# Second MoE of an attention and MoE chain: units of two tiles with 256-column first-layer products and two sets of split second weights

## The reference

```python
logits = x @ w_gate                       # 3072 x 8
expert_idx = np.argmax(logits, axis=1)
probs = softmax(logits)
gate_w = probs[np.arange(N), expert_idx]
for e in range(E):                        # E = 8
    mask = expert_idx == e
    xe = x[mask]
    h = np.maximum(xe @ w1[e], 0.0)       # 512 -> 1024
    ye = h @ w2[e]                        # 1024 -> 512
    out[mask] = gate_w[mask, None] * ye
```

## Time and profile before

| | us |
|---|---|
| median of 3 runs (lowest, highest) | 483.22 (481.46, 484.78) |
| the profiled execution, device time | 484.04 |
| its span, first to last instruction | 482.3 |
| PE busy | 454.6 (94%) |
| DVE busy | 235.2 (49%) |
| ACT busy | 226.3 (47%) |
| POOL busy | 203.1 (42%) |

### The profile page before, as it was taken

One profiled execution on the slowest core, in us unless ns is written; L12 is line 12 of the kernel. 1 busy time (PEld: TensorE's weight loads), 2 busy tenths in 40 slices (PEclk: granted clock), 3 DMA queues, 4 the chain that ended last, 5 costly groups with the idle time before them and its releaser, 6 DMA issues. The chain is left out here.

```text
span 482.3 us, 9916 instructions
## 1 busy us (share of the span) xinstructions
PE 454.6 (94%) x3215; PEld 380.6 (79%) x3216; DVE 235.2 (49%) x760; ACT 226.3 (47%) x455; POOL 203.1 (42%) x179
## 2 busy tenths in 40 slices
PE   8899999999999979989999997999999999999972
PEld 7689999999999976734445864788888888888852
DVE  6567777777777743453210685423333332333352
ACT  2588778878788625321100007333344343334441
POOL 3998888888888100101000000043333333333322
PEclk9999999999999989997998979899999999999977
DMA  8699898976772139479991094511111111111111
GB/s 247 262 419 365 316 378 319 362 246 221 260 256 82 47 98 410 196 269 389 399 408 63 6 379 151 180 54 54 38 49 54 49 54 54 54 40 47 51 29 28
DMA packets 27156, 89.06 MB, mean 185 GB/s; under 512 B 3248, under 2 KB 3248, under 8 KB 27120
## 3 DMA queue, kind: packets, MB, share of 16 engines
q1 hardware_dynamic: 23664, 78.47, 43.9%
q0 software_dynamic: 3296, 9.70, 6.0%
q10 hardware_dynamic: 160, 0.42, 0.4%
HBM read 80.72 MB, written 8.13 MB: 184 GB/s over the span
## 5 line engine op out<-in xcount | busy, mean ns | idle before, releaser
L438 ACT ACTIVATE Pb<-Pb,nm 128x256 f32<-128x256 f32 (+1 forms) x192 | 83.9, 486 | 32.8 <-DVE nm L541 32.8
L381 PE MATMUL O<-V,PTs 128*128 128x65 f32 x704 | 90.1, 269 | 1.0 <-ACT PTs L464 1.0
L1357 PE MATMUL Gp<-w2h,hh 128*128 128x512 f32 x200 | 85.2, 426 | 5.3 <-DVE w2l L1573 3.5
L381 PEld LDWEIGHTS O<-V,PTs 128*128 128x128 f32 x704 | 86.5, 191 | 2.3 <-ACT PTs L464 1.6
L541 DVE CUSTOM_DVE_ANT_0 Pb<-S,TA 128x256 f32<-128x256 f32 (+1 forms) x192 | 68.8, 396 | 37.1 <-PE S L354 34.6
L1358 PE MATMUL Gp<-w2l,hh 128*128 128x512 f32 x200 | 80.0, 400 | 0.0
L1359 PE MATMUL Gp<-w2h,hl 128*128 128x512 f32 x200 | 79.9, 400 | 0.0
L1391 ACT ACTIVATE hh<-Gp 128x512 fp32r<-128x512 f32 x51 | 30.6, 600 | 89.9 <-PE Gp L1297 88.2
L313 POOL TENSOR_TENSOR kl<-k_raw,kh 128x1632 fp32r<-128x1632 f32 x15 | 55.2, 3677 | 9.3 <-ACT kh L448 9.1
L1243 POOL DMA_INDIRECT Cg<-c_rows,src x25 | 24.6, 984 | 77.5 <-PE Cp L1290 75.7
L1597 DVE TENSOR_SCALAR mem<-Gp,gate_s 128x512 f32 x25 | 18.8, 751 | 76.3 <-DMA out<-mem,dst 72.4
(11 more groups left out here) (219 smaller groups left out, 645.0 us busy)
## 6 DMA issues: line engine op xcount, KB each, us to landing
mem<-in_moe_w SPq DMA_DIRECT2D x14, 2048.0 KB, 11.8
ext<-in_moe_w SPq DMA_DIRECT2D x6, 2048.0 KB, 19.3
k_raw<-in_k SPq DMA_DIRECT2D x15, 816.0 KB, 7.7
q_raw<-in_q SPq DMA_DIRECT2D x15, 768.0 KB, 6.0
V<-in_v SPq DMA_DIRECT2D x16, 715.0 KB, 5.9
c_rows<-XL POOLq DMA_DIRECT2D x1, 1536.0 KB, 13.8
k_raw<-in_k ACTq DMA_DIRECT2D x2, 204.0 KB, 4.8
Cg<-c_rows,src POOLq DMA_INDIRECT x25, 2.6
```

The source lines that it names most:

```text
L381: mm = pe.matmul(O[grp % 2][:, at:at + VC], PTs[:, par, (h * kbs + kb) * P:(h * kbs + kb + 1) * P], V[:, buf, h, vb, :], start=(n == 0), s ...
L438: nc.scalar.activation(Pb[:, par, h, 0:width(g)], Pb[:, par, h, 0:width(g)], ACT.Exp, bias=nm[:, par, h:h + 1], scale=-1.0).then_inc(exp_d ...
L1357: pe.matmul(Y, hh[:, fc, :], w2h[:, cols], start=(fc == 0), stop=False)
```

## The change

A rank's tiles are now taken in units of two tiles (256 tokens): rank 0 has 12 units, rank 1 has 1 unit, of which the second tile is empty. PE runs both tiles of each unit, so 26 tiles' second layers; POOL scatters only the 25 real ones. `MAXT`, the width of the routing tables, goes from 34 to 42.

- First layer: one `hidden(u+1)` for each unit, 8 products of 256 columns into all four banks of `Gp`; results go to two banks of their own, `Yq`. It stands behind the first tile's second layer. `turn` transposes two tiles, and ACT copies 256 columns of `CgT`.
- relu and remainder run in four quarters of 512 columns (2 steps fc by 256 tokens); `hh` and `hl` share memory with the routing tables in `work`.
- `w2h` and `w2l` exist twice, set by `rank & 1`. SP loads the second weights of ranks 0 and 1 straight into the two `w2l` right after the first weights, and both are split in place ahead of the loop (`high_in_place`, `rest_in_place`). Each rank's end splits the weights of the rank two later, if there is one, else one idle chunk.
- POOL issues two gathers for each unit ahead of its scatters.
- The memory of x (`xmem`) is given back before the stage, and `CT` moves onto `Cn`, for which ACT waits for `c4_done` in the soft MoE.

```diff
-MAXT = TT + NE + 2
+MAXU = TT // 2 + NE + 1
+MAXT = 2 * MAXU
@@ soft_moe, ACT
                 act.wait_ge(ct_turned, 1)
+                act.wait_ge(c4_done, 1)
@@ top1_moe
-    w2h = sb(st, "w2h", [P, WSIZE], F32R)
-    w2l = sb(st, "w2l", [P, WSIZE], F32R)
+    w2h = sb(st, "w2h", [P, 2, WSIZE], F32R)
+    w2l = sb(st, "w2l", [P, 2, WSIZE], F32R)
@@ SP
             load_v1(sp, entry(sp, odd, 0), odd)
+        for r in range(2):
+            load_v2(sp, entry(sp, r, 0), w2l[:, r, :].bitcast(F32), v2_loaded[r])
         used = count(sp)
-        load_v2(sp, entry(sp, 0, 0))
@@ PE
-        def hidden(u, half):
+        def hidden(u):
             pe.wait_ge(cgt_out, u + 1)
-            pe.wait_ge(g_here[half], u + 1)
-            for fc in range(half * 4, half * 4 + 4):
-                mm = pe.matmul(Hq[half][:, (fc % 4) * P:(fc % 4 + 1) * P],
+            pe.wait_ge(g_here, u + 1)
+            for fc in range(FC):
+                mm = pe.matmul(Gp[:, fc // 2, fc % 2 * 2 * P:(fc % 2 + 1) * 2 * P],
                                Gst[:, fc * P:(fc + 1) * P], CgT[:], start=True, stop=True)
-            mm.then_inc(hid_done, 1)
+                if fc % 2:
+                    mm.then_inc(hid_done, 1)
@@ ACT, ahead of the loop
-        turned_out(0)
-        fetch(0, 0)
-        second_high(0)
-        fetch(0, 1)
-        relu(0, 0)
-        fetch(e1, 0)
-        for ch in range(1, W2CH):
-            second_high(ch)
+        turned_out(0)
+        fetch(0)
+        high_in_place(0, 0)
+        for q in range(4):
+            relu(0, q)
+            if q < 3:
+                high_in_place(0, q + 1)
+        fetch(e1)
+        for ch in range(W2CH):
+            high_in_place(1, ch)
@@ DVE, in the loop
-                low(u, 1)
-                low(u + 1, 0)
...
+                scaled(0)
+                for q in range(3):
+                    low(u + 1, q)
+                scaled(1)
+                low(u + 1, 3)
```

More of the change, by code:

```diff
@@ L1145, in top1_moe, with column, unit @@
     st.enter_context(block)
[L1147 to L1149 removed]
+    def column(t):
+        return t if isinstance(t, int) else t.with_bounds(min_val=0, max_val=MAXT - 2)
+    def unit(u):
+        return u if isinstance(u, int) else u.with_bounds(min_val=0, max_val=MAXU - 1)
     def rank_at(r):
@@ L1250, in _ @@
         pool.wait_ge(dst_ready, 1)
[L1251 to L1265, removed]
+        used, total = count(pool), all_tiles(pool)
+        with pool.Fori(0, used) as rank:
+            units, first = entry(pool, rank, 1), entry(pool, rank, 2)
+            tiles, tile0 = entry(pool, rank, 3), entry(pool, rank, 4)
+            with pool.Fori(0, units) as j:
+                u = first + j
+                gather(u + 2, u + 2)
+                with pool.Fori(0, 1 + (tiles > j * 2 + 1)) as i:
+                    done = tile0 + j * 2 + i
+                    pool.wait_ge(row_free, u * 2 + i + 1)
+                    pool.sem_inc(pool_step, 1)
+                    nc.gpsimd.tensor_copy(dst1[:], dst_i[:, bass.ds(column(u * 2 + i), 1)]).then_inc(dst_copied, 1)
+                    pool.wait_ge(dst_copied, done + 1)
+                    pool.wait_ge(y_scaled, u * 2 + i + 3)
+                    pool.sem_inc(pool_step, 1)
+                    nc.gpsimd.indirect_dma_start(
+                        out=out_d, out_offset=bass.IndirectOffsetOnAxis(ap=dst1[:, 0:1], axis=0),
+                        in_=Ysb, in_offset=None, bounds_check=TOK - 1, oob_is_err=False
+                    ).then_inc(stored, 16)
         pool.wait_ge(stored, total * 16)
         pool.sem_inc(pool_step, 1)
-        pool.wait_ge(gathered, (total + 3) * 16)
+        units = all_units(pool)
+        pool.wait_ge(gathered, (units + 2) * 32)
         pool.sem_inc(pool_step, 1)
@@ L1339, in _ @@
         pe.wait_ge(g_low, pairs_of(used) * 4 + 2)
-        for half in range(2):
-            hidden(0, half)
+        hidden(0)
         pe.wait_ge(rt_ready, 1)
         with pe.Fori(0, used) as rank:
-            tiles, first = entry(pe, rank, 1), entry(pe, rank, 2)
-            with pe.Fori(0, tiles) as j:
+            units, first = entry(pe, rank, 1), entry(pe, rank, 2)
+            high, low = [w[:, bass.ds(rank & 1, 1), :].rearrange("p a f -> p (a f)") for w in (w2h, w2l)]
+            with pe.Fori(0, units) as j:
@@ L1421, in _ @@
-        for ch in range(1, W2CH):
-            second_high(ch)
+        fetch(0)
[7 more added lines that the diff above has]
+            high_in_place(1, ch)
         with act.Fori(0, used) as rank:
-            tiles, first = entry(act, rank, 1), entry(act, rank, 2)
-            with act.Fori(0, tiles) as j:
+            units, first = entry(act, rank, 1), entry(act, rank, 2)
+            with act.Fori(0, units) as j:
@@ L1426, in _ @@
                 u = first + j
-                ahead = [expert(u + 1), expert(u + 2)]
-                relu(u, 1)
-                fetch(ahead[0], 1)
+                ahead = expert(u + 2)
                 turned_out(u + 1)
-                relu(u + 1, 0)
-                fetch(ahead[1], 0)
-            act.wait_ge(v2_loaded, (rank + 1 + (rank + 1 < used)) * 16)
-            act.sem_inc(act_passed, 1)
-            with act.Fori(0, chunks_after(rank, used)) as ch:
-                act.wait_ge(y_half, (first + tiles) * 2 + 1 + (ch >> 1))
-                act.sem_inc(act_passed, 1)
-                nc.scalar.copy(w2h[:, chunk(ch)], raw[:, chunk(ch)]).then_inc(w2_high, 1)
+                act.wait_ge(hid_done, u * 4 + 8)
@@ new lines, in _ @@
+                act.sem_inc(act_passed, 1)
+                fetch(ahead)
+                for q in range(4):
+                    relu(u + 1, q)
+            act.wait_ge(v2_loaded[1], (rank + 1) * (rank + 2 < used) * 16 + 16)
+            act.sem_inc(act_passed, 1)
+            act.wait_ge(y_quarter, (first + units) * 4 + 4)
+            act.sem_inc(act_passed, 1)
+            with act.Fori(0, chunks_at_end(rank, used)) as ch:
+                nc.scalar.copy(w2h[:, bass.ds(rank & 1, 1), chunk(ch)].rearrange("p a f -> p (a f)"),
+                               raw[:, chunk(ch)]).then_inc(w2_high, 1)
@@ L1584, in _ @@
         step(v.tensor_tensor(gate_s[:], sf[:, 1, :], Sp[:, 2 * MAXT:3 * MAXT], ALU.add))
+        for ch in range(W2CH):
+            rest_in_place(1, ch)
         with dve.Fori(0, used) as rank:
[L1586 to L1587 removed]
+            units, first, tile0 = entry(dve, rank, 1), entry(dve, rank, 2), entry(dve, rank, 4)
+            with dve.Fori(0, units) as j:
                 u = first + j
[L1589 to L1598 removed]
```

277 lines of the change are left out of this document (150 added, 127 removed).

## The result

The changed kernel takes 467.82 us (median of 4 runs, 467.25 to 469.34), the kernel before in the same session 483.62. The ratio is 0.9683 with a 95% interval of 0.9641 to 0.9725: 3.2% faster. In a later session it was 0.9696 (0.9670 to 0.9722). The profiled execution has a span of 466.4 us against 482.3, so there are 15.9 us to account for.

What follows compares the result with a forecast made beforehand. PE was taken to bound the loop, busy 20.00 of 20.00 us at full clock. Span 482.3 - 9.7 (loop) - 5.4 (expert change and tail) + 1.0 (start) = 468.2, then + 1.7 - 0.8 gives 469.1 us; range 464.5 to 475.

Steps and rivals of the forecast that it cites:

- The loop: First layer in 256-column products: 0.97 us instead of 1.78 a pair, unit 12.17 us, 9.7 us saved over 12 units.
- Its comparison: Price of a 128-column first-layer product in the kernel before, 0.39 / 4 = 0.098 us, as lower bound for 256 columns.
- Register work costs nothing: First tile of a unit: PE's address computations, some 1.2 us, costed at nothing because the sequencer runs ahead.
- The scatter chain inside a unit: Scatter landing, second scaling, last remainder: slack 2.3 us before DVE is late, 5 us before PE is.
- The start: Ahead of the first second-layer product: wider tables +0.6 us, then ACT and DVE work; together +1.0 us.
- Behind the first product: Unit 0 at half clock: DVE needs 1.9 us a quarter, PE 2.8, so no wait; no change in time counted.
- The thinnest cover: End of unit 0's first tile: ACT's CgT copy at 309.6, PE wants it at about 310; cover 0.4 us.
- The change of expert and the tail: Last unit to end: 3.5 us wait and half clock go, POOL's drain ends at S+16.8 instead of S+22.2; 5.4 saved.
- 256 columns at twice the price: Rival in the first layer: 0.195 us a product, saving only 0.15 a unit, total 477.7 us; chance 0.06.
- the sequencer's work: Rival in each unit's first tile: register work shows, 13 units x 1.2 = 15.6 us, total 484.7; chance 0.03.
- The start did not pay: Rival at unit 0: late CgT, second-set load or gathers hold PE 2 to 3 us plus clock, 472 to 475; chance 0.17.
- The slower one: Rival in the loop: landing wait holds PE; decides above 1.1 us a unit, 498 us at a 10 us landing; chance 0.03.

Runs made afterwards that it cites:

- The experiment: Changed kernel with the first layer of a unit as sixteen 128-column products in one group instead of eight of 256: 479.79 us, ratio 0.9917.
- the filler: Changed kernel plus nine unused 128-column fp32 products on PE behind the first hidden(0), in the wait ahead of the loop: 468.57 us, ratio 0.9712.
- the second run: Changed kernel with the second expert's weights split at the end of the first expert instead of ahead of the loop: 474.14 us, ratio 0.9815.
- the runs on the empty tile: Changed kernel with PE making 6 products instead of 24 for the last unit's empty tile: 469.66 us, ratio 0.9731.

## Why the prediction was right, point by point

467.8 us were measured and 469.1 forecast. Spans are compared here, 466.4 measured against 468.2. That the sum is so near is in part luck: the loop gave 0.4 us more than forecast, the tail 1.3 less and the start 2.7 more, and most of that last is the state of the clock in one execution.

- **The loop** (9.7 us forecast, 10.1 measured). The unit came out at 12.14 us against 12.17. The group of eight cost 0.95 us against 0.97: 0.119 a product where I had 0.115 from the attention, and no seam where I had 0.05. The attention's row could be carried over: what both share is a weight load for each product. That the load is what costs is argued only.
- **Its comparison** was mis-sized. From groups of four I took 0.098 us for a 128-column product; in a row of sixteen it is 0.109, and the attention's rows of 0.11 to 0.12 could have been read before. The sum didn't use this number by itself, only the group with its seam, 0.44, so the saving held. The experiment's expectation did use it and was 3 us short.
- **Register work costs nothing**: confirmed, 0.23 us between products with and without it. The instruction that took 0.102 us in the earlier trace rows takes 0.046 here.
- **The scatter chain inside a unit**: right for PE, with less to spare at first. DVE waited for a landing four times before 334 us, up to 3.7 us, because 2.77 us of issue stood on POOL ahead of the first scatter (314.34). Once a late landing reached PE: the last remainder of unit 1 ended at 319.00 and its product started at 319.24, 0.09 us late. From 339 us to the last unit DVE's scalings wait for PE alone.
- **The start** (+1.0 forecast, -0.1 at the first product, and -1.6 behind it). This step failed, in two ways. The first is a clock that the sum took as it was in one profile. The wider tables cost DVE 0.2 us each as counted (1.21 against 1.01), and from the stage's first DVE instruction to the first product of the sort it is 14.17 us (267.20 to 281.37) against 13.53, 0.6 more, as forecast. But then PE did the sort in 4.00 us instead of 4.55, and the first group of G products took 3.14 us against 3.64; the granted clock was 0.91 from 280 to 298 us against 0.81. That need not be the change's doing, for it differs between executions of the same code: in the run without the last gather, whose code is the same up to here, the sort took 4.80 us. The sort before, in the changed kernel, and in that run:

```profile
280.61 4.55 PE L1283 MATMUL Sp<-OW,OB 128*128 128x34 f32 x24 [0.85 <-DVE OB L1520]
...
281.37 4.00 PE L1311 MATMUL Sp<-work 128*128 128x42 f32 x24 [1.48 <-DVE work L1564]
...
279.83 4.80 PE L1312 MATMUL Sp<-work 128*128 128x42 f32 x24 [1.46 <-DVE work L1565]
```

In that run it is 34.83 us from the stage's first DVE instruction to the first second-layer product (265.68 to 300.51), in the changed kernel 33.73 and before 33.96. So with the sort as slow as before the change costs 0.9, near the forecast 1.0; that the changed kernel's profile had its first product early is luck.

- **Behind the first product**, the second way: I had counted no change, and two tiles took 15.22 us to the turn (steady: 12.14 + 1.4) where they had taken 17.69 (301.04 to 318.73; steady: 12.98 + 1.4): an excess of 1.7 instead of 3.3. PE's timeline of before shows what the 3.3 were: 2.4 us of half clock (twelve products and a turn in 5.31 us, 301.04 to 306.35, for 2.86 at the loop's pace), 0.3 for a DVE remainder that ended at 306.92, and 0.4 at the turn of 312.16, which waited for a gather. Now about seven products run at half clock and neither wait is there. How much of the shorter half clock the change brought is open: in the second profile of the changed kernel the stretch took 15.48 us at a clock of 0.72 (298 to 310 us) instead of 0.86, and the kernel before was profiled once.
- **The thinnest cover** was named rightly and was thinner: 0.1 us at 308.2 where I had 0.4 at 309.6. With the filler it was gone.
- **The change of expert and the tail** (5.4 forecast, 4.1 measured). The wait and the half clock went, as forecast; the second run puts about 4 us on them. The step that was mis-sized is POOL's chain: I had the last scatter at S+8.6, and it came at S+10.1 (458.46, with S = 448.32). The rows show the terms: 2.54 us of register loads at the change of rank, 0.85 behind the first index copy, 1.01 behind the second, and 0.30 between the two gathers. DVE's scaling was held by its own loads as well (3.01 us of issue). That is 1.5 us late, and the drain itself took 0.17 more. A third error took back 0.6: I had the drain begin 3.7 us behind the scatter's start, and it began 3.1 behind it (461.6); before it was 2.7 (474.96 to 477.7), so the earlier trace rows would have given less. With 0.2 from the drain's end to the span's end that makes the 1.3 us. That POOL's drain and not PE or DVE ends the kernel was right, and the runs on the empty tile and on the last gather show it from both sides.
- **The rivals**: 256 columns at twice the price fell (0.119 against 0.109), and so did the sequencer's work (no gaps). The start did not pay: the cover held by 0.1 us. The slower one, the scatter chain, cost PE 0.09 us in the loop; the same chain decides the end.

## What to carry to other kernels

Where each product has a weight load of its own, look whether a wider moving side costs more at all: widening it from 128 to 256 columns was worth nearly half of the first layer here (0.95 us against 1.74 for a unit), and grouping alone was worth nothing. When a kernel ends with a scatter, follow the issuing engine's queue back from it: what stands ahead of the last scatter sets the end, and work of another engine under it is free, here a whole empty tile, until that queue is shortened. Work that is moved ahead of a loop lengthens the chain of the engine that takes it, so look there for the next bound before filling PE's gaps. And before reading the start or the end of two profiles against each other, take off what was different already ahead of the edit; here that was up to 2.6 us.

## What the runs showed of the hardware

- Pitch of fp32r products with a weight load each, at 2.4 GHz: 0.109 us at 128 columns in a row of sixteen, 0.098 in groups of four between 512-column products, 0.119 at 256 columns, 0.228 at 512.
- POOL's drain behind the last scatter took 4.57 and 4.40 us, and it began 3.1 and 2.5 us behind the start of that scatter (458.46 to 461.6, 456.39 to 458.9).
- A granted clock of 1.00 in place of 0.50 over some seven products changed no time (15.22 us both), since another engine's chain was as long. With that chain shorter and the half clock there it was 15.18.
- The granted clock of the same code differed between executions: the sort took 3.63 to 4.96 us in the profiles of the changed kernel and its variants.
